# Attention tiles in plain fp32 beside two gated MLPs: halves side by side in the array, one operation per tile

## The reference

```
# q, k, v: (B=2, H=8, S=768, D=40); gates i, f: (B, H, S); o: (B, H, S, D)
for t in range(S):                       # gated linear attention with a stabiliser
    m_new = max(f[t] + m, i[t])
    C = exp(f[t] + m - m_new) * C + exp(i[t] - m_new) * outer(v[t], k[t])
    n = exp(f[t] + m - m_new) * n + exp(i[t] - m_new) * k[t]
    y[t] = sigmoid(o[t]) * (C q[t]) / max(|n q[t]|, 1);  m = m_new
x = y as (1536 tokens, 320)
x = (silu(xn @ w_gate) * (xn @ w_val)) @ w_out      # xn = x / rms(x) * rms_g, width 1536
x = (sigmoid(x @ w_gate2) * (x @ w_val2)) @ w_out2  # width 1536
```

## Time and profile before

| | us |
|---|---|
| runs of the kernel, median of 3 | 537.92 (534.52 to 542.44) |
| the profiled execution | 539.07 |
| its span, first to last instruction | 537.3 |
| PE busy in it | 498.7 |
| DVE busy | 252.6 |
| ACT busy | 199.5 |
| mean granted TensorE clock | 0.956 |

### The profile page before, as it was taken

One profiled execution on the slowest core, in us unless ns is written; L12 is line 12 of the kernel. 1 busy time (PEld: TensorE's weight loads), 2 busy tenths in 40 slices (PEclk: granted clock), 3 DMA queues, 4 the chain that ended last, 5 costly groups with the idle time before them and its releaser, 6 DMA issues.

```text
span 537.3 us, 7236 instructions
## 1 busy us (share of the span) xinstructions
PE 498.7 (93%) x2604; PEld 413.5 (77%) x2604; DVE 252.6 (47%) x532; ACT 199.5 (37%) x406; POOL 27.5 (5%) x50
## 2 busy tenths in 40 slices
PE   7976787795998899999999999999999999999996
PEld 4666777795986788888788888888888888888884
DVE  6473585876664664654464545422232222322222
ACT  6352453544442443432454446421232212322122
POOL 2310010011111010000000000000000000000000
PEclk9685797999899999999999999999999999999999
DMA  7239472165425223140013231000001000010001
GB/s 185 69 90 244 126 207 61 42 169 159 141 86 144 69 71 101 54 137 1 1 58 121 84 117 38 1 1 1 0 0 50 1 1 0 1 49 1 0 1 49
DMA packets 20630, 36.70 MB, mean 68 GB/s; under 512 B 2930, under 2 KB 11570, under 8 KB 20594
## 3 DMA queue, kind: packets, MB, share of 16 engines
q1 hardware_dynamic: 20082, 36.05, 23.1%
q10 hardware_dynamic: 512, 0.18, 0.2%
HBM read 23.27 MB, written 1.97 MB: 47 GB/s over the span
## 4 chain that ended last, share of the span: by engine, by line
PE 81%; issue 9%; DVE 4%; DMA 2%; ACT 2%; SPq 1%; POOL 1%; ACTq 0%; POOLq 0%; DVEq 0%
PE bank L1233 48%; PE bank L1284 6%; PE bank L1285 6%; PE bank L1286 6%; PE bank L1187 3%; PE bank L1293 3%; PE bank L1292 3%; PE bank L1133 2%; PE bank L1207 1%; DMA swap_raw<-qk 1%; PE bank L1175 1%; PE bank L1193 1%; DMA qk_st<-qk_parts 1%; PE bank L1156 1%; PE bank L1221 1%
## 5 line engine op out<-in xcount | busy, mean ns | idle before, releaser
L1233 PE MATMUL bank<-x_hi,gv_split 128*128 128x512 f32 (+1 forms) x800 | 252.0, 383 | 8.5 <-DVE hid L981 4.9
L1233 PE MATMUL bank<-x_lo,gv_split 128*128 128x512 f32 (+1 forms) x480 | 180.6, 379 | 0.0
L1233 PEld LDWEIGHTS bank<-x_hi,gv_split 128*128 128x128 f32 x800 | 150.5, 195 | 38.7 <-issue 5.0
L1233 PEld LDWEIGHTS bank<-x_lo,gv_split 128*128 128x128 f32 x480 | 93.6, 195 | 16.2
L596 ACT ACTIVATE hid_hi<-hid 128x512 fp32r<-128x512 f32 (+1 forms) x80 | 47.1, 588 | 156.5 <-DVE hid L994 93.2
L994 DVE TENSOR_TENSOR hid<-hid,bank 128x512 f32<-128x512 f32 x48 | 33.0, 687 | 139.5 <-PE bank L1233 139.5
L589 ACT ACTIVATE hid<-bank 128x512 f32<-128x512 f32 (+1 forms) x80 | 44.2, 552 | 114.0 <-PE bank L1233 113.9
L1001 DVE TENSOR_TENSOR hid_lo<-hid,hid_hi 128x512 fp32r<-128x512 f32 (+1 forms) x80 | 51.2, 640 | 38.6 <-ACT hid_hi L596 37.8
L1284 PE MATMUL bank<-hid_hi,wo_split 128*128 128x512 f32 (+1 forms) x160 | 61.8, 386 | 3.5 <-DVE hid_lo L1001 1.9
L1285 PE MATMUL bank<-hid_lo,wo_split 128*128 128x512 f32 (+1 forms) x160 | 60.7, 379 | 0.0
L1286 PE MATMUL bank<-hid_hi,wo_split 128*128 128x512 f32 (+1 forms) x160 | 60.4, 378 | 0.0
(11 more groups left out here) (136 smaller groups left out, 438.7 us busy)
## 6 DMA issues: line engine op xcount, KB each, us to landing
qk_st<-qk_parts SPq DMA_DIRECT2D x60, 160.0 KB
gv_raw<-wgv SPq DMA_DIRECT2D x12, 384.0 KB, 3.2
swap_raw<-wgv SPq DMA_DIRECT2D x12, 384.0 KB, 4.7
wo_raw<-wo SPq DMA_DIRECT2D x24, 160.0 KB, 3.2
qk_raw<-qk SPq DMA_DIRECT2D x6, 480.0 KB, 5.7
v_sb<-v SPq DMA_DIRECT2D x12, 168.0 KB, 3.6
gate<-og SPq DMA_DIRECT2D x12, 160.0 KB, 4.1
k_sb<-k SPq DMA_DIRECT2D x10, 160.0 KB, 3.6
```

The source lines that it names most:

```text
L1233: mm = pe.matmul(ps[:, 0:size], lhs, rhs, start=(i == 0), stop=(i == len(passes) - 1))
```

## The change

The split of q, k and state is gone, with its copies. A tile's q and k are loaded as they are, one half in partitions 0 to 39 and the other in 64 to 103 (`load_qk`, three buffers). `scores` and the state part of `outputs` are plain fp32 products of 40 rows, the two halves in turn; the state of the two halves lies in the same two row ranges, and `state_sums` writes it with 64 columns per half (k is padded for that). Exponents, exponential, weighing, and combining are one operation for a whole tile, in two adjoining PSUM banks that hold in turn the arguments, the scores and the outputs. The mean square moves from DVE to POOL. The gain of the norm, formerly in the split of the weights, is put on x (`round_x`, `rest_x`, three operations each instead of one), and `rest_gv` is one operation instead of two or three. k, v and raw w_out have three buffers instead of two.

The schedule is new: SPLIT is 6, which makes 78 units; tiles 2 and 3 get their exponents in units 0 and 2, tiles 4 to 11 in units 9 to 26. The scores come after the result products, the outputs after the value products. The weights are prepared in units 0 to 3 and 9 to 14, w_out a unit later. The third part of the gate rows is spread over units 3 to 7 (`G2`). In the prologue DVE begins the second part of the gate rows before it weighs the scores, ACT makes one of the four spreads, the transposes of tiles 0 and 1 stand ahead of the gates' own, and there are 33 fillers.

The core of the diff (the removed functions are printed above; every loop of the other engines follows the tables at its head):

```diff
-SPLIT = 8
+SPLIT = 6
...
-OUT_AT = {u + 1: j for u, j in SCORE_AT.items()}
-NORM_AT = {u: j // 2 for u, j in OUT_AT.items() if j % 2}
-TURN_AT = {u + 1: t for u, t in NORM_AT.items()}
-SUM_AT = {0: 0, 2: 1, **{u: t for u, t in NORM_AT.items() if t < NT - B}}
-
-PREP_AT = {**{f - 2: f for f in range(2, SPLIT)}, **{SPLIT + f - 4: f for f in range(SPLIT, NF)}}
+SCORE_AT = dict(zip([0, 2, 9, 11, 13, 15, 18, 20, 23, 26], range(B, NT)))
+EARLY_TURN = 7
+OUT_AT = {u + 1: t for u, t in SCORE_AT.items()}
+TURN_AT = {u + (2 if t < EARLY_TURN else 1): t for u, t in OUT_AT.items()}
+SCALE_AT = {u - (t < EARLY_TURN): t for u, t in TURN_AT.items()}
+PREP_AT = {**{f - 2: f for f in range(2, SPLIT)}, **{SPLIT + f - 3: f for f in range(SPLIT, NF)}}
...
-WARM = (10, 2, 1, 0, 0, 0, 0, 9, 8, 5, 6)
+G2 = (3, 4, 5, 6, 7)
+WARM = (12, 0, 0, 0, 0, 14, 3, 4)
...
-            qk_parts = sba("qk_parts", [GROUP * D, 4, HG, L], F32R)
-            qk_hi, qk_lo = qk_parts[:, 0::2], qk_parts[:, 1::2]
+            qk = [sba(f"qk_tile{i}", [P, 2, HG, L]) for i in range(3)]
-            v_sb = [sba(f"v_sb{p}", [P, H, DV]) for p in range(2)]
+            v_sb = [sba(f"v_sb{p}", [P, H, DV]) for p in range(3)]
...
-            def spread_qk(j):
-
-                (m, i), st = group_of(j), qk_st[j % 4]
-                mine = slice(D * i, D * i + D)
-                sp.wait_ge(qk_split, m + 1)
-                if j >= FIRST + 4:
-                    sp.wait_ge(att_out, j - 3)
-                for part, (q, k) in enumerate(((0, 2), (0, 3), (1, 2))):
-                    sp.dma_start(st[D * part:D * part + D].bitcast(F32),
-                                 qk_parts[mine, q:k + 1:k - q].bitcast(F32)).then_inc(spread_in[j % 4], 16)
+            def load_qk(t):
+                need(sp, s_done, 2 * t - 4)
+                if t - 3 >= B:
+                    sp.wait_ge(att_out, 2 * t - 4)
+                for g in range(2):
+                    sp.dma_start(qk[t % 3][ROWS * g:ROWS * g + D], qk1[2 * t + g]).then_inc(qk_in[t % 3], 16)
...
             def load_k(t):
                 if t < NT - B:
-                    need(sp, st_done, t - 1)
-                    sp.dma_start(k_sb[t % 2][:], k1[t]).then_inc(k_in[t % 2], 16)
+                    need(sp, st_done, t - 2)
+                    sp.dma_start(k_sb[t % 3][:, 0:DM], k1[t].rearrange("l h d -> l (h d)")).then_inc(k_in[t % 3], 16)
...
             def load_wo(n):
-                need(sp, wo_ready, n - 1)
-                sp.dma_start(wo_raw[n % 2][:], (wo1, wo2)[n // NF][n % NF]).then_inc(wo_in[n % 2], 16)
+                need(sp, wo_ready, n - 2)
+                sp.dma_start(wo_raw[n % 3][:], (wo1, wo2)[n // NF][n % NF]).then_inc(wo_in[n % 3], 16)
...
                 load_rows(j)
             load_gv(2)
-            load_wo(2)
-            spread_qk(FIRST)
-            load_k(1)
-            load_v(2)
+            load_gate(2)
+            load_gate(3)
+            load_v(3)
             for u in range(PART1 + 1):
                 gv, out = weight_steps(u + 1)
                 for n in gv:
                     load_gv(n)
...
                 if u in OUT_AT:
-                    j = OUT_AT[u]
-                    t, g = j // 2, j % 2
-                    if g == 0 and t + 1 < NT:
-                        load_v(t + 1)
-                if u == 0:
-                    spread_qk(FIRST + 1)
-                    load_group(1)
-                    load_gate(2)
...
-                            load_group(m + 1)
+                    t = OUT_AT[u]
+                    if t + 2 < NT:
+                        load_qk(t + 2)
+                    if t + 2 < NT:
+                        load_v(t + 2)
+                    load_k(t + 1)
...
+            def fade_state(t):
+
+                pool.wait_ge(state_done, t)
+                nc.gpsimd.tensor_tensor(faded[:], state[t % B][:],
+                                        c_col[:, t, :].unsqueeze(2).broadcast_to([P, HG, DV]),
                                         ALU.mult).then_inc(decayed, 1)
 
             def root(t):
+                pool.wait_ge(ssq_done, t + 1)
+                need(pool, rstd_done, t - 1)
+                nc.gpsimd.tensor_scalar(mine(msq, t), mine(ssq, t), 1.0 / DM, 1e-6, ALU.mult, ALU.add).then_inc(msq_done, 1)
...
+            def exponential(t):
+                act.wait_ge(arg_done, 2 * t + 2)
+                act.wait_ge(att_out, 2 * t - 2)
+                nc.scalar.activation(prob[t % 2][:].rearrange("p g h s -> p (g h s)"),
+                                     pair_ps[:].rearrange("p g c -> p (g c)"), ACT.Exp).then_inc(exp_done, 2)
...
-            def round_state(t):
-                act.wait_ge(state_done, t + 1)
-                act.wait_ge(att_out, 2 * t + 2)
-                nc.scalar.activation(s_st[t % B][0:D], state[t % B][:], ACT.Copy).then_inc(s_rounded, 1)
+                nc.scalar.activation(hsum[:].rearrange("p g h d -> p (g h) d")[:, :, 0:D], gate[t % 2][:], ACT.Square, accum_out=mine(ssq, t)).then_inc(ssq_done, 1)
...
-                                     xt_ps(t)[:, 0:3 * P].rearrange("p (m s) -> p m s", m=3),
-                                     ACT.Copy).then_inc(xhi_done, 1)
+                act.wait_ge(gains_in, 16)
+                for m in range(3):
+                    ins = nc.scalar.activation(x_hi[:, m, bass.ts(t, P)], xt_ps(t)[:, P * m:P * m + P], ACT.Copy,
...
-                need(act, gv_ready, n)
-                nc.scalar.activation(w_tail[:].bitcast(F32R), raw[:, :, 2], ACT.Copy,
-                                     scale=gain_tail[:] if n < NF else tail_w).then_inc(gv_rounded, 1)
+                nc.scalar.activation(wgv[f][:, :, 0:2], raw[:, :, 0:2], ACT.Copy)
+                nc.scalar.activation(wgv[f][:, :, 2], raw[:, :, 2], ACT.Copy, scale=tail_w).then_inc(gv_rounded, 1)
...
             scale_y(1)
             round_x(0)
             round_x(1)
+            gate_exponentials(1)
             round_gv(1)
             for u in range(UNITS):
                 late = u in TURN_AT and u in ENDS
+                early = u in TURN_AT and TURN_AT[u] < EARLY_TURN
                 if late:
...
+            def weigh_scores(t):
+                dve.wait_ge(s_done, 2 * t + 2)
+                dve.wait_ge(exp_done, 2 * t + 2)
+                own = prob[t % 2][:].rearrange("p g h s -> p (g h s)")
+                nc.vector.tensor_tensor(own, pair_ps[:].rearrange("p g c -> p (g c)"), own, ALU.mult).then_inc(p_done, 2)
+
+            def combine(t):
+
+                own = pair_ps[:, :, 0:2 * HG * DV].rearrange("p g (j h d) -> p g j h d", j=2, h=HG)
+                dve.wait_ge(att_out, 2 * t + 2)
+                dve.wait_ge(y1_done, t)
+                dve.wait_ge(ssq_done, t)
+                need(dve, comb_done, t - B)
                 if t % B == 0 and t <= 2 * B:
                     dve.wait_ge(cols_done, t // B + 1)
-                nc.vector.tensor_tensor(inter[:], own[:, 1],
-                                        r_col[:, t, heads].unsqueeze(2).broadcast_to([P, HG, DV]),
-                                        ALU.mult).then_inc(comb_part, 1)
-                dve.wait_ge(comb_part, j - FIRST + 1)
-                nc.vector.tensor_tensor(hsum[:, heads], own[:, 0], inter[:], ALU.add).then_inc(comb_done, 1)
+                nc.vector.tensor_tensor(inter[:], own[:, :, 1],
+                                        r_col[:, t, :].rearrange("p (g h) -> p g h", g=2).unsqueeze(3)
+                                        .broadcast_to([P, 2, HG, DV]), ALU.mult).then_inc(comb_part, 1)
+                dve.wait_ge(comb_part, t - B + 1)
+                nc.vector.tensor_tensor(hsum[:], own[:, :, 0], inter[:], ALU.add).then_inc(comb_done, 1)
...
             def update_state(t):
                 else:
                     dve.wait_ge(decayed, t - B + 1)
-                    nc.vector.tensor_tensor(state[t % B][:], sums, state[t % B][:], ALU.add).then_inc(state_done, 1)
-
...
-                                        xt_ps(t)[:, 0:3 * P].rearrange("p (m s) -> p m s", m=3),
-                                        x_hi[:, :, bass.ts(t, P)].bitcast(F32),
-                                        ALU.subtract).then_inc(xlo_done, 1)
+                for m in range(3):
+                    ins = nc.vector.scalar_tensor_tensor(
+                nc.vector.tensor_tensor(wgv[f][:, :, 3:6], raw[:], wgv[f][:, :, 0:3].bitcast(F32),
+                                        ALU.subtract).then_inc(gv_ready, 1)
...
             weight_rows(1)
             rest_x(0)
             rest_x(1)
+            take_columns(0)
+            decays(1)
             rest_gv(1)
+            take_columns(1)
             for u in range(UNITS):
                 late = u in TURN_AT and u in ENDS
-                if u in TURN_AT:
-                    mean_square(TURN_AT[u])
+                early = u in TURN_AT and TURN_AT[u] < EARLY_TURN
                 if late:
                     rest_x(TURN_AT[u])
                 if u < TANH_UNITS:
...
```

(81 more changed lines are left out.)

501 lines of the change are left out of this document (191 added, 310 removed).

## The result

The changed kernel takes 506.75 us in the median of four runs (503.78 to 512.85), the kernel before 539.69 in four beside it: a ratio of 0.938, with a 95% interval of 0.927 to 0.949. On another chip, six runs against eleven gave 506.24 against 534.88, 0.948 (0.945 to 0.952). It is 5 to 6% faster. The forecast was 509 us, between 493 and 527. The profiled execution has 505.26 us and a span of 503.5.

What follows compares the result with a forecast made beforehand. Before the first full units, in-order queues and waits were taken to cost PE 43 of 111.1 us. 539.07 - 25 - 2 - 3 + 3 = 512, taken as 510 profiled and 509 median; range 493 to 527 us.

Steps and rivals of the forecast that it cites:

- the 43 lost microseconds: Units 0 to 15: 67.5 us of work in 111.1; 18 lost instead of 43 after the change, so -25 us.
- PE's products: Scores, state part and state sums as plain fp32: +0.3 us a tile, 3 us over ten tiles, bounds -5 and +24.
- Weights late: Before the first full units: weights still late once or twice, 4 us, half of the old ACT wait.
- Unit 3's pile and the gate rows: DVE work ahead of gate_hidden(4) in unit 3, 3 us; gate rows slowing units 4 to 7, 4 us.
- Low clock: Before the first full units, after waits: 12 us of work at 1.2 instead of 2.4 GHz, 6 to 7 us more.
- The prologue's -3: Before unit 0: tile 0's mean square and transpose come sooner; 2.6 us taken, bounds 0 and 4.5.
- The later stretch's -2: From the first full units to the last tile: 3 us lost instead of 5.
- Switches of the array: Changes between row and column splits, some six a tile: no pause seen in the trace, nothing charged.
- Rival 3: Array halves don't overlap, or switches drain it: +10 to +21 us, 519 to 530, taken 524; chance 0.09.
- Rival 1: Weights and DVE still pace units 0 to 9, units 3 to 9 at 1.2 GHz: 16 us more, 525; chance 0.17.
- Rival 2: Nearly all waits go: 8 us lost in place of 21, 496 us; chance 0.12.
- Rival 4: PE waits in each tile for exponential, weighing and combining: 4.5 us each over ten tiles, 554 us; chance 0.07.

Runs made afterwards that it cites:

- b_free: Kernel before without the split, copies and stacking of q, k and state; score and state products use a constant tile: 517.03 us against 537.98, 0.961.
- a_copies: Changed kernel plus 100 copies of 96 KB (9.6 MB) inside SBUF that nobody reads: 503.83 us against 537.98, 0.938.
- the second profile: The changed kernel itself, repeated and profiled again beside two versions meant to beat it: 506.24 us, 0.948.
- b_free_dead: b_free with sixty 160 KB copies put back in the old queue places, their result read by nobody: 520.33 us against 538.13, 0.968.
- tuned1: Changed kernel with ACT's last gate rows behind the activation, last_logs differences on POOL, mask rows in unit 3: 504.64 us, 0.942.
- a_rows_once: Changed kernel with the third part of the gate rows in one piece (units 6 and 7): 506.55 us against 538.13, 0.941.
- a_serial: Changed kernel with a tile's two halves one after the other in scores and state part, instead of by turns: 518.67 us against 537.98, 0.963.
- a_halves: Changed kernel with exponential, weighing and combining by halves again: 506.94 us against 538.13, 0.944.
- a_split8: Changed kernel with eight halved blocks (SPLIT 8) instead of six: 511.60 us against 538.13, 0.953.
- b_plain: Kernel before without the split, with real plain fp32 products, both halves in array rows 0 to 39, unpaired: ratio 1.003.
- tuned2: tuned1 with the state sums issued behind a group of result products: 506.07 us, 0.946.

## Why the prediction was right, and where its steps were not

**The place and the mechanism were right.** The gain was to be in the 43 lost microseconds before the first full units, and to come from the split and its waits. b_free alone brings 21.5 us of the 31.5 there, 21 in the median; how much of that is waits and how much the splitting operations themselves is open.

**How much stays lost was too pessimistic.** With PE's products as measured the stretch holds about 69 us of work; 11 are lost, not 18. Three terms made up the 18. Weights late, 4 us: no wait in the list goes back to a transfer, so 0. Unit 3's pile and the gate rows, 7 us: PE was idle for 79.6 - 75.4 = 4.2 us in this profile, but for 6.7 in a_copies and in the second profile, where the clock was at 1.00 and 0.98, so this term was about right. Low clock, 6 to 7 us: at a mean of 0.94 about 12% of the stretch, 9.5 us, ran at 1.2 instead of 2.4 GHz, which loses 4.8; in a_copies it is 0. The two terms trade against each other, and together they came to 9 us and less, not 13. The mark moved by 35.3 us where I had written 25 to 30; without the prologue it is 31.5.

**The number was helped by errors that cancel.** Without the prologue the spans differ by 31.5 - 1.5 = 30 us, where the forecast had 25 + 2 + 3 - 3 = 27. Too little was taken for the first stretch; the prologue's 3 and the later stretch's 2 were no gains of the change.

**The prologue's -3 was wrong in its reason.** I gave it to the mean square and the transpose being made sooner. Unit 0 starts between 23.3 and 24.2 us in some profiles (a_copies 23.28, the changed kernel 23.80 and 24.09, b_free_dead 24.22, the kernel before, second time, 23.83), and between 27.6 and 29.8 in others (the kernel before 27.6, tuned1 27.83, a_rows_once 27.86, b_free 29.81), whichever order the prologue has. It goes with the speed of PE: the mean granted clock before unit 0 is 0.93 in the second profile of before and 0.81 in the first, 0.75 in tuned1. b_free's profile gives 1.00 there, but its steps say otherwise. In PE's timeline of it, sixteen early scores take 2.01 us, to 9.14, in place of 1.10:

```profile
7.13 2.08 PE L1093 MATMUL bank<-hid 40*128 40x128 f32 x16 [1.38 <-DMA hid<-qk]
```

Whether the new order adds something below this scatter stays open.

**The later stretch's -2 did come as idle time, and was lost again.** Up to the last tile PE is idle for 118.1 - 117.2 = 0.9 us, before for 116.4 - 113.3 = 3.1. But the stretch and what is behind it are 1.5 us longer: PE's products take about 2 us more, and the clock of 0.97 (6% of 118 us at half speed) loses 3.5.

**PE's products were nearly right as a sum, by errors that cancel.** Scores: 0.9 taken, 1.09 measured. My reason to go below the 1.10 of the earlier trace rows, that the fillers ahead had run slowly, was false: the granted clock was 1.00 from 7.0 to 8.2 us, and sixteen scores at half speed take the 2.01 us of b_free. State part: 1.0 taken, 1.02 measured. Sums: 0.8, measured 0.60. Outputs: unchanged, measured +0.19, half of it the step from the last output to the first state product. The total was to be +0.3 and is +0.40.

**Switches of the array** were charged at nothing, because the next instruction began before the recorded end of the last 40-row one. That shows nothing, since recorded lengths overlap everywhere (0.28 us against a step of 0.12). The steps show it: between 86.12 and 86.23 the step of a 256-column product is 0.11, and from 86.23 to the scores it is 0.21. About 0.1 us more stands in front of each group of 40-row products, and about 0.2 inside its 1.09 us; for the scores and the state part of a tile I estimate 0.5 us from these steps. It is inside the +0.40. Rival 3 had 0.17 for each of six switches, 1.0 us a tile, and by its size (+10 us) it is refuted: a_serial shows what it takes to lose 12. The Trainium skill's rule that a change of the tiling mode drains TensorE (same page and section as before) is consistent with such gaps, which do not prove it.

**The rivals.** Rival 1 (weights and DVE set the pace) is refuted by the window of rows: no weight is late. Rival 2 (nearly all waits go, 496) came half true: the waits on weights and exponentials went, but some of the clock and the gate rows stayed. Rival 4 (stalls of the tile-wide chain) is refuted: not one PE wait above 1 us on the exponential in the changed kernel, and a_halves is no different.

**What is not settled.** The changed kernel's stretch is 10 us shorter than b_free's (79.6 against 89.6), although PE's products are dearer. SPLIT 6 explains about 5 (a_split8, with the new order). For the other 5 or more, the moved exponents, the third w_out buffer, the single operation for weights and the removed copies of the mean square are left together; the whole-tile operations and the spread of the gate rows are excluded by their runs. No run took the new order alone. Nor did one keep the splitting operations of ACT and DVE without the copies and their waits.

## What to carry to other kernels

Price a transfer by who waits for it in order, and not only by its bytes: here the split of q, k and state cost 21 us, of which the bytes of its 9.6 MB of copies alone brought back 3 by the medians (8 in one first stretch, through weights that came late), and nothing in an order with room for the weights. The other 18 were the queues behind them and the splitting operations together. Before going from split products to plain fp32 ones of few rows, see that two row ranges can be served by turns: without turns the price was 12 us, and in one range alone 23, the whole gain of leaving out the split. And read at least two profiles of the same kernel before giving the change a few microseconds of its prologue.

## What the runs showed of the chip that I had not expected

**Few rows are not cheap, turns are.** An instruction of a plain fp32 product of 40 rows steps at 0.11 us, like one of 128 rows (b_plain, and its outputs). By turns in two row ranges a pair takes that 0.11 us. Around a group of them stand some 0.1 us in front and 0.2 inside, which is why eight in one range take 1.09 us (0.136 each) and sixteen in two blocks 1.64. The moving columns hardly matter (128: 1.09 us for sixteen by turns; 42: 1.02). The clock does: at half speed, in b_free's prologue, the sixteen take 2.01 us.

**The clock fell with PE never idle.** In the timeline of the changed kernel, after 3.4 us of narrow products (outputs, state part, sums) the products from 111.00 on step at 0.43 us instead of 0.23: 1.2 instead of 2.4 GHz, up to 114.50, with no idle time ahead. The same is seen from 46.3 to 49.7 and from 80.4 to 83.8, and from 213.5 to 216.9 behind 2.8 us of outputs and state part alone, but not behind every tile. a_copies had a clock of 1.00 through all of its first stretch with the same products, and fell in the same way later, at 125.3 and 190.1 us. The cause is open; tuned2 broke up that run and the falls stayed.
